# Exponents of the local attention taken tile by tile with the maximum as bias, one weight split moved ahead, and the head's transfers in another order

## What is computed

```python
def _attn_ref(q, k, v):                       # 4 batches, 8 heads, 576 tokens, head size 64
    q_d, k_d, v_d = (mean over groups of 4 tokens of q, k, v)
    out_d = sm_attn(q_d, k_d, v_d)            # full attention over the 144 pooled tokens
    out_up = np.repeat(out_d, 4, axis=2)
    mask = np.abs(pos[:, None] - pos[None, :]) < 4
    scores = np.where(mask, scale * q @ k.T, -1e9)
    scores = scores - np.max(scores, axis=-1, keepdims=True)
    attn = np.exp(scores)
    attn = attn / (np.sum(attn, axis=-1, keepdims=True) + 1e-09)
    return out_up + attn @ v

def _moe_ref(x, w_gate, w_val, w_out):        # 2304 tokens, 512 -> 1536 -> 512
    return (sigmoid(x @ w_gate) * (x @ w_val)) @ w_out

# _moe2_ref: soft routing of the result over 8 experts with 4 slots each (phi, w1, w2)
```

## Time and profile before

| | us |
|---|---|
| median of three runs | 590.64 (589.9 to 591.19) |
| the profiled execution | 588.38 |
| its span | 586.6 |
| PE busy | 547.7 (93% of the span) |
| DVE busy | 224.3 (38%) |
| ACT busy | 200.1 (34%) |
| POOL busy | 103.2 (18%) |

### The profile page before, as it was taken

The page is one execution under the profiler, slowest core; times in us unless marked ns, Lnnn a source line. Parts: engine busy times, 40 slices in busy tenths (PEclk is TensorE's granted clock), DMA queues, the critical chain, the costliest instruction groups (busy, mean ns, idle before and its releaser), DMA issues.

```text
span 586.6 us, 11364 instructions
## 1 busy us (share of the span) xinstructions
PE 547.7 (93%) x4530; PEld 412.6 (70%) x4530; DVE 224.3 (38%) x500; ACT 200.1 (34%) x514; POOL 103.2 (18%) x171
## 2 busy tenths in 40 slices
PE   6676998999999999999999999999999999999983
PEld 5555776777778768777777778787787777865432
DVE  3896851444625252434325253542212221041103
ACT  3664654434243333242333234233213121231113
POOL 7864022141231202121120302110000000000000
PEclk9998999999999999999999999999999999999997
DMA  7677932121220211111020210101702347599958
GB/s 177 157 170 223 334 92 58 44 73 32 65 72 13 59 25 41 43 42 43 21 62 3 58 27 22 24 2 29 280 1 84 132 164 263 180 404 394 399 207 322
DMA packets 86708, 70.98 MB, mean 121 GB/s; under 512 B 61312, under 2 KB 65920, under 8 KB 86656
## 3 DMA queue, kind: packets, MB, share of 16 engines
q1 hardware_dynamic: 86656, 70.25, 38.2%
HBM read 65.52 MB, written 4.72 MB: 120 GB/s over the span
## 4 chain that ended last, share of the span: by engine, by line
PE 86%; DVE 4%; DMA 2%; SPq 2%; issue 1%; ACT 1%; POOL 1%; POOLq 0%; DVEq 0%
PE gateb L962 27%; PE valb L962 25%; PE unitb L972 5%; PE unitb L915 3%; PE unitb L1062 3%; PE gateb L1081 2%; PE unitb L871 2%; PE unitb L878 2%; PE unitb L986 2%; PE unitb L1011 2%; PE unitb L906 2%; PE unitb L886 2%; PE unitb L893 1%; PE unitb L899 1%; PE unitb L921 1%
## 5 line engine op out<-in xcount | busy, mean ns | idle before, releaser
L962 PE MATMUL gateb<-w_hl,xhl 128*128 128x512 f32 x648 | 163.5, 401 | 0.0
L962 PE MATMUL valb<-w_hl,xhl 128*128 128x512 f32 x648 | 161.8, 399 | 0.0
L962 PEld LDWEIGHTS gateb<-w_hl,xhl 128*128 128x128 f32 x648 | 119.1, 190 | 33.2 <-issue 8.9
L962 PEld LDWEIGHTS valb<-w_hl,xhl 128*128 128x128 f32 x648 | 118.6, 188 | 23.4 <-issue 0.2
L672 ACT ACTIVATE hid<-gateb 128x512 f32<-128x512 f32 x54 | 32.3, 598 | 171.1 <-PE gateb L962 171.1
L792 DVE SCALAR_TENSOR_TENSOR hid<-hid,valb 128x512 f32<-128x512 f32 x54 | 37.1, 686 | 126.3 <-PE valb L962 126.3
L590 POOL TENSOR_TENSOR vd<-v 72x256 f32<-72x256 f32 x16 | 12.9, 806 | 163.6 <-PE unitb L899 162.4
L601 ACT ACTIVATE hT<-unitb 128x512 f32<-128x512 f32 x54 | 32.0, 597 | 21.2 <-PE unitb L972 21.2
L972 PE MATMUL unitb<-ident,hid 128*128 128x128 f32 x216 | 33.3, 278 | 2.5 <-DVE hid L792 1.7
L775 DVE TENSOR_TENSOR xraw<-unitb,outd 128x192 f32<-128x192 f32 x43 | 15.0, 356 | 53.6 <-PE unitb L915 53.4
L972 PEld LDWEIGHTS unitb<-ident,hid 128*128 128x128 f32 x216 | 24.3, 140 | 7.7 <-issue 4.1
(11 more groups left out here) (176 smaller groups left out, 667.9 us busy)
## 6 DMA issues: line engine op xcount, KB each, us to landing
ew_low<-in_moe_w_dram SPq DMA_DIRECT2D x19, 1024.0 KB, 11.9
ew_high<-in_moe_w_dram SPq DMA_DIRECT2D x13, 1024.0 KB, 7.5
qtok<-in_q_dram SPq DMA_DIRECT2D x32, 144.0 KB, 2.7
ktok<-in_k_dram SPq DMA_DIRECT2D x32, 144.0 KB, 3.2
v<-in_v_dram SPq DMA_DIRECT2D x32, 144.0 KB
out_dram<-outs SPq DMA_DIRECT2D x18, 256.0 KB, 3.0
vloc<-in_v_dram SPq DMA_DIRECT2D x32, 112.0 KB
xraw<-in_moe_w_out_dram SPq DMA_DIRECT2D x12, 256.0 KB, 5.7
```

What stands on the lines that cost most here:

```text
L962: last = mm(bank[:, :], xhl[:, i % NX, x, kk, :], w_hl[:, c, m, w, kk, :], start=j == 0, stop=j == len(order) - 1)
```

## The change

The mask is added and the scores are scaled in one instruction, so that `prob` holds scores on the final scale. The maxima are stored negated. The subtraction over 630 columns is gone: `ex` is now nine Exps of 70 columns, each with its column of `mx` as bias and each giving the row sum of its block into `sm`, and so `norm` no longer takes the sums. The first weight piece is split one turn earlier, ahead of `mx0` of pair 0, so that five pieces and not four are split in the head. The middle part of local v comes in two transfers of 70 windows, no longer in four. SyncE issues the first weight piece ahead of the pieces of `w_out`, and puts the loads for the pairs 4 and 5 behind all weight pieces.

```diff
-               """WT S0+ S1+ WT GP GP mx0+ mx1+ ex+ Sd+ pool_V+ Q++ mxd+ exd+ K++""",
+               """WT S0+ S1+ WT GP GP w_hi w_lo mx0+ mx1+ ex+ Sd+ pool_V+ Q++ mxd+ exd+ K++""",
...
             for h in range(2):
-                body_rows = mid[h][key_start(1):key_start(1) + QT * (NQ - 2), :].rearrange("(t r) d -> r t d", r=QT)
-                sp.dma_start(vloc[0:QT, 1:NQ - 1, h, :], body_rows).then_inc(v_in, 16)
-                over = mid[h][key_start(1) + QT:key_start(1) + QT * (NQ - 1), :].rearrange("(t r) d -> r t d", r=QT)
-                sp.dma_start(vloc[QT:KW, 1:NQ - 1, h, :], over[0:KW - QT]).then_inc(v_in, 16)
+                windows = bass.AP(tensor=mid.tensor, offset=mid.offset + (h * S + key_start(1)) * D,
+                                  ap=[[D, KW], [QT * D, NQ - 2], [1, D]])
+                sp.dma_start(vloc[:, 1:NQ - 1, h, :], windows).then_inc(v_in, 16)
...
             elif name == "ex":
-                act.wait_ge(sub_done, arg + 1)
-                nc.scalar.activation(prob[:, arg % 2, :, :], prob[:, arg % 2, :, :], ACT.Exp, scale=SCALE / SCALE_D)\
-                    .then_inc(exp_done, 1)
+                act.wait_ge(max_done, 2 * (arg + 1))
+                wait(act, sum_step, 2 * arg)
+                for t in range(NQ):
+                    last = nc.scalar.activation(prob[:, arg % 2, t, :], prob[:, arg % 2, t, :], ACT.Exp,
+                                                bias=mx[:, t:t + 1], accum_out=sm[:, t:t + 1])
+                last.then_inc(exp_done, 1)
...
-                nc.vector.tensor_tensor(prob[:, arg % 2, t0:t1, :],
-                                        ub[:, 0:(t1 - t0) * KW].rearrange("p (t n) -> p t n", n=KW),
-                                        mask[:, t0:t1, :], ALU.add).then_inc(free, 1)
+                wait(dve, exp_done, arg)
+                nc.vector.scalar_tensor_tensor(out=prob[:, arg % 2, t0:t1, :],
+                                               in0=ub[:, 0:(t1 - t0) * KW].rearrange("p (t n) -> p t n", n=KW),
+                                               scalar=SCALE / SCALE_D, in1=mask[:, t0:t1, :],
+                                               op0=ALU.mult, op1=ALU.add).then_inc(free, 1)
                 wait_free(dve, unit)
-                nc.vector.reduce_max(mx[:, t0:t1], prob[:, arg % 2, t0:t1, :], AX.X).then_inc(max_done, 1)
-                if u == 1:
-                    dve.wait_ge(max_done, 2 * arg + 2)
-                    nc.vector.tensor_tensor(prob[:, arg % 2, :, :], prob[:, arg % 2, :, :],
-                                            mx[:, :].unsqueeze(2).to_broadcast([P, NQ, KW]),
-                                            ALU.subtract).then_inc(sub_done, 1)
+                nc.vector.reduce_max(mx[:, t0:t1], prob[:, arg % 2, t0:t1, :], AX.X, negate=True).then_inc(max_done, 1)
...
-                nc.vector.reduce_sum(sm[:, :], prob[:, arg % 2, :, :], AX.X).then_inc(sum_step, 1)
...
+        put_off = [("pool_V", HP - 1), ("Q1", HP), ("K1", HP)]
...
             load_pair_qk(sp, 0, "k")
+            load_pieces(sp, range(0, 1))
             for f in range(2):
                 load_wo_piece(sp, f)
...
             for s in head:
-                sync_step(sp, s)
+                if s not in put_off:
+                    sync_step(sp, s)
...
+            for s in put_off:
+                sync_step(sp, s)
```

More of the change, by code:

```diff
@@ L747, in dve_step @@
                 dve.wait_ge(exp_done, arg + 1)
[L748 to L749 removed]
                 nc.vector.tensor_scalar(sm[:, :], sm[:, :], EPS, None, ALU.add).then_inc(sum_step, 1)
[L751 removed]
+                dve.wait_ge(sum_step, 2 * arg + 1)
                 nc.vector.reciprocal(inv[:, :], sm[:, :]).then_inc(sum_step, 1)
[L753 removed]
+                dve.wait_ge(sum_step, 2 * arg + 2)
                 nc.vector.tensor_tensor(prob[:, arg % 2, :, :], prob[:, arg % 2, :, :],
@@ L1178, in _ @@
                 if s == ("S1", 0):
-                    load_pieces(sp, range(0, 2))
+                    load_pieces(sp, range(1, 3))
                 if s[0] == "PV2" and s[1] < 2:
-                    load_pieces(sp, range(s[1] + 2, s[1] + 3))
+                    load_pieces(sp, range(s[1] + 3, s[1] + 4))
                 if s == ("PV2", 2):
-                    load_pieces(sp, range(4, 6))
+                    load_pieces(sp, range(5, 6))
                     for f in range(2, 6):
@@ L1221, in _ @@
                         part = mask[h * QT:(h + 1) * QT, t0:t1, :]
-                        nc.gpsimd.affine_select(out=part, in_=part, compare_op=ALU.is_ge, fill=MASKED / SCALE * SCALE_D,
+                        nc.gpsimd.affine_select(out=part, in_=part, compare_op=ALU.is_ge, fill=MASKED,
                                                 base=-least if sign > 0 else least + 6,
```

6 lines of the change are left out of this document (1 added, 5 removed).

## The result

| | before | after |
|---|---|---|
| median, us | 590.91 (589.9 to 591.64, 4 runs) | 612.39 (610.59 to 614.07, 4 runs) |
| profiled execution, us | 588.38 | 610.59 |
| its span, us | 586.6 | 608.8 |
| mean granted clock of TensorE | 0.987 | 0.971 |

The change makes the kernel slower: the ratio is 1.0362, 95% interval 1.0337 to 1.0388, some 21 us. The forecast was 600.7, so the direction was right, and the loss was twice the one forecast (21.5 for 10). The time lies above the range too.

What follows compares the result with a forecast made beforehand. VectorE was taken to bound the head and TensorE the body. Span 586.6 + 2.9 (head) + 7.2 (body) = 596.7; the difference of +10.1 on the median 590.64 gave 600.7 us, range 593.0 to 604.5.

Steps and rivals of the forecast that it cites:

- The price of the Exps: ScalarE's local softmax: 0.33 us for each Exp, 2.97 for nine, 2.36 more for each pair than the one Exp.
- The rival with 0.25: Exps on ScalarE at the Trainium skill's 0.25 us each, body loses 3.7 us, head level: 594.3 us, chance 0.20.
- The waits of the body: TensorE waiting for banks ScalarE frees behind the Exps: 1.8, 1.8, 2.4, 0.6, 0.6 for pairs 5, 6, 7, 11, 4; +7.2 us.
- the upper bound of 8.3: Body: the loss in us from TensorE's waits with the Exp at its highest price, 0.36 us.
- The moved split: Head's start: VectorE's first scores at 16.2 us instead of 9.60, `norm_d` of pair 0 ending at 25.3 instead of 18.9.
- The turns: Head: 10.9, 9.87 and 9.87 us between ends of `norm_d`, ScalarE working nearly throughout; pair 3's ends at 56.0 instead of 49.62.
- The head's end: Last `norm_d` to first gate: 4.4 us instead of 6.9, the 2.47 wait for local v gone; first gate at 61.1.
- The rival that had the first gate fall to 1.2 GHz again: Head's end: TensorE's clock falls all the same, so 1.7 us do not come back; 602.4 us, chance 0.15.
- The put-off at nothing: Later loads for pairs 4 and 5 cost nothing: q of pair 5 lands near 69, wanted not before 72 us.
- the step that took TensorE's clock as given: Body: the added waits of TensorE counted at their length, +7.2 us, with no slow clock behind them.
- the slow clock of the first turn: Head's first turn: TensorE idles some 8 us, so 0.7 us added for its small products at the lower clock.

Runs made afterwards that it cites:

- warm_all: The kernel after with filling transposes at the body's three waits (pairs 4 to 6) and idle-time matmuls on TensorE in the head; 602.6 us, ratio 1.0213.
- fill_all: The kernel after with the first two transpose units of pairs 4, 5 and 6 done four times over, body only; 607.06 us, ratio 1.0264.
- vloc_only: The kernel before with local v in four transfers instead of six and nothing else; 591.34 us, ratio 0.9991.
- best_warm: The kernel before with local v in four transfers, the late loads put off, and idle-time matmuls on TensorE in the head; 588.28 us, ratio 0.9964.

## Why the prediction was right and wrong

- **The price of the Exps** was right: 0.33 us forecast, 0.34 measured. The rival with 0.25 falls. The Trainium skill's figure (ScalarE: Activation LUTs, What ACT_TABLE_LOAD costs), from which that rival came, doesn't agree with this trace, which has a read of the accumulator behind each Exp.
- **The waits of the body** were right one by one: 1.8, 1.8 and 2.4 forecast, 1.8, 1.9 and 2.4 more than before measured, and 0.7 for pair 11 (0.6). Pair 4's place cost 0.5 in the two kernels with the body's waits filled (0.6). A wait of 1.3 us for the halves of x at 312 us, behind the Exps of another pair, was costed at nothing. With the body's waits filled it lost 9.4 us (warm_all: delay 4.5 at val(0,0), 13.9 at the end), 1.1 above the upper bound of 8.3 and 2.2 above the forecast.
- **The moved split** was mis-sized by 2 us in the profile of the kernel after: scores at 18.2 and not 16.2. TensorE's unit on the first w_out piece started 2.5 us later than before, where the sum delays the `GP` copy by 1.0, and the split took 1.78 and not 1.25. By the end of `norm_d` it was 3 us, 28.3 for 25.3, with the transposes ahead of it at half speed. The other kernels with this start had the w_out unit at 8.6 to 10.4, the scores at 16.4 to 18.7 and that end at 25.3 to 28.8, and the 25.3 is of the kept-busy kernel. So the forecast was the best case of a landing that varies.
- **The turns** were right for TensorE at full clock: 10.9, 9.6 and 10.2 measured in the kept-busy kernel (warm_all), 10.9, 9.9 and 9.9 forecast. In the other kernels with nine Exps in the head they took up to 12.3 us.
- **The head's end** was right in its shape: no wait for v, the first gate at full clock, 4.0 us from the last `norm_d` to it (4.4 forecast). The 4.0 is a good case: other kernels with nine Exps took 5.0 to 7.1. Waits of 0.8 and 1.1 us for v, in earlier turns, were not in the sum. The rival that had the first gate fall to 1.2 GHz again (602.4) was nearer in time, but by another mechanism: that gate took 2.97 us.
- **The put-off at nothing** was right within what can be told.
- **What failed is the step that took TensorE's clock as given.** The prediction used the row of 0.66 between 50 and 60 us and the gate of 4.44 us for the head's end, had a rival for that one gate, and gave 0.7 us to the slow clock of the first turn. It put the clock behind the other waits that it added at nothing, without a reason: three places in the body where TensorE stands still for 1.8 to 2.7 us, two of them shortly behind another wait of 1.5. It did not see the waits for K's copy in the turns of the head at all (2.6 and 1.5 us in the profile of the kernel after, three of 2.6 in several other kernels with nine Exps there). The forecast of +10 us became +12.4 in the kernel kept busy (602.6 against 590.17), of which some 2 us are the filling's own, and +21.5 without. The range contains the former. Of the difference 5.3 to 5.8 us are the body's (fill_all, by medians and by ratios) and 3 to 4.5 the head's (warm_all against fill_all, measured at different times, so known to 2 us or so).

What stays open: the executions of one kernel differ in where in the head the clock falls, and I have no account of which waits bring it down and which don't. A single wait of 1.49 us that ended at 91.5 us left the clock at 1.00 in the profile of before and was followed by a `val` of 4.26 us in that of vloc_only, whose body is the same. Nor does its length decide. In the head of the kernel after the wait for K's copy left the clock alone, timeline and stretch:

```profile
36.52 1.32 PE L877 MATMUL unitb<-kT,qT 64*64 64x70 f32 x36 [2.64 <-ACT kT L600]
...
30.00:40.00 10.00, 7.01 (x119) 5.94 (x119) 7.18 (x15) 8.65 (x34) 6.57 (x9) 1.00 0.56 99
```

In fill_all the same wait of 2.63 was followed by a clock of 0.50 from 37 to 40 us. The profile of the kernel after is its fastest execution. Its first gate starts at 63.33, that of fill_all, which differs only in the body, at 65.17.

## What to carry to other kernels

A new wait on TensorE is not worth its own length alone. Where the profile already shows a stretch under 1.00 behind an idle one, price each added wait a second time with the units behind it at half speed, as a case with a chance of its own, and price removing one the same way. On an engine that feeds TensorE by small copies, one operation of 0.6 us and nine of 0.34 are different things, even if the engine has time to spare over the whole stretch: ask what is queued behind the whole block, at each place where the block stands. Where a wait can't be removed, repeated work in its bank is a cheap way to find out how much of the loss is clock, as long as the filling doesn't itself run at the low clock and hold up what stands behind it.

## What the runs showed of the hardware

- More work made the kernel faster: 54 transposes more, spread over three places, and 5.3 us less (612.39 to 607.06); with 38 small matmuls more in the head 9.8 us less (to 602.6). A `val` of 12 matmuls of 512 columns took 3.0 us in the filled places and 4.5 to 5.4 in the others.
- TensorE stood still for 2.64 us ahead of 36.52 and the clock stayed at 1.00 (kernel after); it stood still for 1.45 us ahead of 114.84 and the clock was at 0.50 from 117 to 119 (best_warm).
- A rounding subtraction of 1024 columns on VectorE took 1.23, 1.31 and 1.78 us at the same place of three kernels, and 1.25 on average before.
- In the kernel after SyncE took 2.7 us to issue the four transfers of one local v ahead of the last weight loads (56.18 to 58.87), and 6.3 us for the same four right behind them (64.86 to 71.13).
